# Values stored with their columns of ones, and a wait ahead of the second piece of keys

## The chip, the cores and the metric

The kernel runs on one core of one Trainium2 chip. The metric is the device time of one execution in microseconds; lower is better.

## The reference, cut to what matters

```python
B, N, C, n_agents, d_ff = 2, 12480, 128, 49, 2048
def sm(a, b):
    s = scale * (a @ b.transpose(0, 2, 1))
    e = np.exp(s - s.max(-1, keepdims=True))
    return e / (e.sum(-1, keepdims=True) + 1e-09)
agent_v = sm(agents, k) @ v                  # (B, 49, 128)
x = (sm(q, agents) @ agent_v).reshape(B * N, C)
h = x @ w_in                                 # (24960, 2048)
out = (np.maximum(h, 0.0) + alpha * np.minimum(h, 0.0)) @ w_out
```

Agents attend to all keys, queries attend to the agents, and a two-layer network with a leaky activation follows. All inputs are float32.

## The kernel before, in words

Five engines follow programs written out by hand, and semaphores alone order them. SyncE (SP in the rows) issues nearly all transfers, in the order of its program: where it waits, every later transfer waits too.

**Before the main loop** the keys and values of batch 0 are gone through. The keys come as a short tail tile `k_tail` and 12 full pieces of 1024 keys (`load_keys`, 512 KB each, one row of 4096 bytes a partition) into eight slots of `kv_s`. A slot has 4 * 257 + 1 = 1029 numbers a partition. TensorE scores each piece against the agents (`piece_scores`, line 480; 16 matmul records a piece), ScalarE saves the scores into `S`, VectorE takes maxima. Then GpSimd subtracts the maximum and ScalarE takes exp, piece by piece. After that TensorE multiplies the exps with the values (`first_values`, line 557; again 16 records a piece). The values come as 12 pieces of 8 tiles of 128 x 128 (`load_values`, line 289) into the same slots, once the keys there have been used.

A matmul of exps with 129 columns, one of them ones, gives the weighted sum and the denominator together. So a slot holds, for each pair of tiles, a one and then 256 numbers of values, and a last one at its end (RUN = 257). In the kernel before, the values lie in device memory without ones. The transfer puts four runs of 1024 bytes into each partition, between the ones (`without_ones`), and VectorE writes the ones (memsets on lines 1307, 1327, 1335 and 1388). TensorE waits for them (`ones_in`, `second_ones`).

**Behind the values** TensorE scores `k_tail` of batch 1, sums denominators, scores `first_keys` (first keys of batch 1), and turns the agents' values into mixed weights. From about 60 us on a loop over 49 chunks of 512 queries runs the network (lines 650, 667 and 677), and the keys and values of batch 1 are worked in between (`second_values` from chunk 12 on, six loads of 1 MB, `load_second`).

The order of SyncE's queue in the first 50 us: `k_tail`, six pieces of keys, `w_out`, six pieces of keys, `w_inT`, `w_in`, the first queries, `v_tail`, value piece 1, queries, value pieces 2 to 12, `k_tail` of batch 1, `first_keys`, queries, and then the transposes of the first chunk (PT<-stack). Value piece 1 waits for key piece 8 to be scored, value piece 5 for all keys, value piece m over 8 for value piece m - 8 to be used.

Of the kernel before, what the change touches and what calls it, by code (L numbers as in the profile page):

```python
# [11 lines left out]
B, N, C, A, F = 2, 12480, 128, 49, 2048  # L12
# [40 lines left out]
def build(nc, kT, kTail, vP, vS, vTail, qT, agT, w_in, w_inT, w_out, alpha_col, out):  # L53
    ctx = ExitStack()
    with ctx:
# [3 lines left out]
        def sem(name):  # L59
            return ctx.enter_context(nc.semaphore(name))  # L60
# [108 lines left out]
        in_q = [sem("in_q0"), sem("in_q1")]  # L169
        stored = [sem("stored0"), sem("stored1")]  # L170

        consts, stack_zero, ones_in, second_ones = sem("consts"), sem("stack_zero"), sem("ones_in"), sem("second_ones")
        pool_step, dve_step = sem("pool_step"), sem("dve_step")
        sel_ready, signs, lin_w_in, relu_w_in = sem("sel_ready"), sem("signs"), sem("lin_w_in"), sem("relu_w_in")
        signs_out, w_signed = sem("signs_out"), sem("w_signed")
# [72 lines left out]
        def value_slot(m):  # L248
            return (m + RING - 1) % (2 * RING)
# [3 lines left out]
            at = t // 2 * RUN + t % 2 * VC  # L253
            return slice(at, at + VC)


        def without_ones(x):
            return x.rearrange("p (j c) -> p j c", c=RUN)[:, :, 1:RUN]

        second_s = kv_s[:, RING:2 * RING, :].rearrange("p s c -> p (s c)")  # L260
        SECOND_SLOT = SECOND // 2 * RUN + 1

# [7 lines left out]
        @block.sync  # L270
        def _(sp):
            def load_keys(m):
                s = (m - 1) % KEY_SLOTS
                if m > KEY_SLOTS:

                    sp.wait_ge(k_scored, m - KEY_SLOTS + 1)
                sp.dma_start(kv_s[:, s, 0:PIECE], kT[0, m - 1]).then_inc(in_k[s], 16)

            def load_values(m):
                if m == 1:  # L280

                    sp.wait_ge(k_scored, KEY_SLOTS + 1)
                if m == RING + 1:

                    sp.wait_ge(k_scored, FULL + 1)
                if m > 2 * RING:

                    sp.wait_ge(v_used, m - 2 * RING + 1)
                sp.dma_start(without_ones(kv_s[:, value_slot(m), 0:4 * RUN]),
                             vP[m - 1].rearrange("p (j c) -> p j c", c=2 * C)).then_inc(in_v[(m - 1) % (2 * RING)], 16)  # L290

            def load_tail(b):
                sp.dma_start(v_tail[:, b, 1:RUN], vTail[b]).then_inc(in_vt[b], 16)

            sp.dma_start(k_tail[:, 0, :], kTail[0]).then_inc(in_kt[0], 16)
            for m in range(1, FULL + 1):
                load_keys(m)
                if m == 6:
                    sp.dma_start(w_lin[:, :, :], w_out).then_inc(in_wo, 16)
            sp.dma_start(w_inT_s[:, :, :], w_inT).then_inc(in_wT, 16)  # L300
            sp.dma_start(w_in_s[:, :], w_in).then_inc(in_wn, 16)
            sp.dma_start(q_s[:, 0, :], qT[0]).then_inc(in_q[0], 16)
            load_tail(0)
            load_values(1)
            sp.dma_start(q_s[:, 1, :], qT[1]).then_inc(in_q[1], 16)
            for m in range(2, FULL + 1):
                load_values(m)

            sp.dma_start(k_tail[:, 1, :], kTail[1]).then_inc(in_kt[1], 16)
            sp.dma_start(first_keys[:, :], kT[1, 0]).then_inc(in_first, 16)  # L310

            def load_queries(n):

                sp.wait_ge(q_scored, n - 1)
                sp.dma_start(q_s[:, n % 2, :], qT[n]).then_inc(in_q[n % 2], 16)

            load_queries(2)

            def load_second(half, j):
                sp.dma_start(without_ones(second_slot(half)[:, 0:SECOND // 2 * RUN]),  # L320
                             vS[j].rearrange("p (j c) -> p j c", c=2 * C)).then_inc(in_second[half], 16)


            def turn(n, half, read=None):

                parts = n - 1
                if not isinstance(n, int):
                    parts = sp.compute_val(parts)

                sp.wait_ge(stack_zero, 1)  # L330
                if read is not None:

                    sp.wait_ge(lin_ready, parts)
                sp.wait_ge(q_hi, n + 1)
                sp.wait_ge(q_dup, n + 1)
                sp.wait_ge(q_lo, n + 1)
                for t in range(4):
                    sp.dma_start(PT[:, half, t * WIDE:(t + 1) * WIDE], stack[:, t, :], transpose=True).then_inc(q_turned, 16)

            def spread(n, half):  # L340

                sp.wait_ge(q_turned, 64 * n + 64)
                for g in range(32, 128, 32):
                    sp.dma_start(PR[g:g + 32, half, :], PT[0:32, half, :]).then_inc(q_spread, 16)

            turn(0, 0)
            load_queries(3)
            spread(0, 0)

            sp.wait_ge(v_used, 2 * RING + 1)  # L350
            for h in range(2):
                sp.dma_start(kv_s[:, h, 0:PIECE], kT[1, EARLY + h - 1]).then_inc(in_k[h], 16)
            load_tail(1)
            turn(1, 1)
            spread(1, 1)

            def body(i, b, kind):
                for half in range(2):
                    n = 2 * i + half
                    if not there(n):  # L360
                        break
                    if there(n + 4):

                        sp.wait_ge(q_scored, n + 3)
                        sp.dma_start(q_s[:, half, 0:width(n + 4)], qT[n + 4][:, 0:width(n + 4)]).then_inc(in_q[half], 16)
                    if kind == KEYS and (not isinstance(n, int) or n + 2 + EARLY <= FULL):

                        sp.wait_ge(k_scored, n + (FULL + EARLY + 2))
                        sp.dma_start(kv_s[:, half, 0:PIECE], kT[1, n + (EARLY + 1)]).then_inc(in_k[half], 16)
                    if kind == TOP:  # L370

                        sp.wait_ge(v_used, FULL + 1)
                        load_second(half, half)
                    if kind == VALUES and (not isinstance(n, int) or n + 2 - FIRST_VALUES < SECONDS):

                        sp.wait_ge(v_used, n + (FULL + 2 - FIRST_VALUES))
                        load_second(half, n + (2 - FIRST_VALUES))
                    if there(n + 2):
                        turn(n + 2, half, n)
                        spread(n + 2, half)  # L380
                    if there(n + 1):

                        sp.wait_ge(y_ready, n + 1)
                        sp.dma_start(out[n], y[:, half, :]).then_inc(stored[half], 16)
                    else:

                        sp.wait_ge(last_y, 1)
                        sp.dma_start(out[n][:, 0:LAST // 2], y[:, half, 0:LAST // 2]).then_inc(stored[half], 16)

            each_body(sp, body)  # L390

            sp.wait_ge(stored[0], 16 * BODIES + 16)
            sp.wait_ge(stored[1], 16 * BODIES + 16)
# [83 lines left out]
        def _(pe):  # L477
# [63 lines left out]
            def first_values(m):  # L541
# [2 lines left out]
                    pe.wait_ge(in_vt[0], 16)  # L544
                else:
                    pe.wait_ge(in_v[(m - 1) % (2 * RING)], 16 * ((m - 1) // (2 * RING) + 1))

                pe.wait_ge(ones_in, RING + 1 if m <= RING else 2 * RING + 1)
                pe.wait_ge(k_exped, m + 1)
                for t in range(count):  # L550
                    if m == 0:
# [252 lines left out]
            def body(i, b, kind):  # L804
                for half in range(2):
# [33 lines left out]
                        pe.wait_ge(in_k[half], 16 * i + 16 * (FULL // KEY_SLOTS + 2))  # L839
                    if kind == VALUES:  # L840
                        pe.wait_ge(in_second[half], 16 * i + 16 * (1 - FIRST_VALUES // 2))

                        pe.wait_ge(second_ones, 2)

                        pe.wait_ge(k_exped, n + (FULL + 2 - FIRST_VALUES))
                        second_values(half)
# [300 lines left out]
        def _(dve):  # L1147
# [156 lines left out]

            dve.memset(stack[:, :, :], 0.0).then_inc(stack_zero, 1)

            dve.memset(v_tail[:, :, 0:RUN + 1:RUN], 1.0).then_inc(ones_in, 1)

            dve.wait_ge(consts, 4)
            for g in (0, 64):  # L1310
                for at, lo, hi in ((0, 0, A), (A, 0, A), (2 * A, REST, A), (128, 0, REST)):
# [3 lines left out]
            for m in range(FULL + 1):  # L1315
# [4 lines left out]
                if m == 9:  # L1320
                    dve.wait_ge(relu_w_in, 1)
                    dve.tensor_reduce(w_col[:, 0:1], w_relu[:, :, :], AX.XY, ALU.max,
                                      apply_absolute_value=True).then_inc(relu_col, 1)
                if m == KEY_SLOTS:

                    for s in range(RING, KEY_SLOTS):
                        dve.memset(kv_s[:, s, 0:4 * RUN + 1:RUN], 1.0).then_inc(ones_in, 1)
            key_max_column(0)
            relu_max_top()
            key_max_diagonal(0, K_BANK)  # L1330
            key_max_save(0, K_BANK)

            dve.wait_ge(k_scored, FULL + 1)
            for s in range(RING):
                dve.memset(kv_s[:, s, 0:4 * RUN + 1:RUN], 1.0).then_inc(ones_in, 1)
            weight_scale()
            query_shift(0)

# [39 lines left out]
            def body(i, b, kind):  # L1378
                for half in range(2):
# [2 lines left out]
                        break  # L1382
                    g = 2 * PAIRS * i + PAIRS * half
                    if kind == TOP and half == 0:

                        dve.wait_ge(v_used, FULL + 1)
                        for h in range(2):
                            dve.memset(second_slot(h)[:, 0:SECOND_SLOT:RUN], 1.0).then_inc(second_ones, 1)

                        dve.wait_ge(b_turned, 1)  # L1390
                        dve.memset(av_rows[:, :], 0.0).then_inc(av_added, 1)
# [106 lines left out]
```

## Time and profile before

| | us |
|---|---|
| median of 3 runs | 900.53 (900.29 to 901.55) |
| the profiled execution, its own time | 901.17 |
| its span in the trace | 899.4 |
| TensorE busy | 892.1, 99% of the span |
| VectorE busy | 619.2, 69% |
| ScalarE busy | 502.4, 56% |

The span is the stretch from the first to the last instruction; the execution's own time has 1.8 us more around it. PE is TensorE's matmuls, PEld its weight loads, DVE is VectorE, ACT is ScalarE, POOL is GpSimd, SPq is SyncE's queue. TensorE is busy nearly all the time, so what matters are its few idle stretches, and who ends them.

### The profile page before, as it was taken

What the parts mean: (1) busy time and instruction counts of PE and PEld (TensorE: products, weight loads), DVE (VectorE), ACT (ScalarE), POOL (GpSimd) and SP (SyncE); (2) the same over time, 40 slices, a digit from 0 to 9 for tenths busy, and PEclk for the clock granted to TensorE, in tenths of its full rate; (3) what the DMA queues carried; (4) which work ended last, traced back from release to release, by engine and by line L of the source; (5) the groups of instructions that cost most, each with busy time, mean ns of one, the idle gap of its engine ahead of it and who ended that gap; (6) DMA issues with size and microseconds to landing.
All of it is one profiled execution on the core that took longest, in us unless ns stands there. A gap on an engine that the chain in (4) does not pass through costs nothing.

```text
span 899.4 us, 15332 instructions
## 1 busy us (share of the span) xinstructions
PE 892.1 (99%) x5496; PEld 451.9 (50%) x5496; DVE 619.2 (69%) x883; ACT 502.4 (56%) x653; POOL 105.5 (12%) x130
## 2 busy tenths in 40 slices
PE   9999999999999999999999999999999999999998
PEld 9855555555544545444444444444444444444444
DVE  4877767766776667678666676667667676766664
ACT  2445565555555555565555566556565655665554
POOL 6500010001000100010001001011010010010100
PEclk9999999999999999999999999999999999999999
DMA  9952223122322341111112112111111121121110
GB/s 358 359 155 82 62 64 103 58 63 69 98 83 85 98 130 43 39 45 53 36 39 62 35 40 61 35 41 58 38 42 54 39 56 38 39 61 33 30 36 21
DMA packets 69975, 66.13 MB, mean 74 GB/s; under 512 B 36368, under 2 KB 54192, under 8 KB 69552
## 3 DMA queue, kind: packets, MB, share of 16 engines
q1 hardware_dynamic: 69504, 65.45, 23.9%
q8 instruction: 25, 0.41, 0.2%
q10 hardware_dynamic: 432, 0.16, 0.1%
q14 instruction: 14, 0.11, 0.0%
HBM read 41.54 MB, written 12.78 MB: 60 GB/s over the span
## 4 chain that ended last, share of the span: by engine, by line
PE 96%; DMA 2%; DVE 1%; ACT 0%; issue 0%; SPq 0%; DVEq 0%; ACTq 0%
PE ps L677 57%; PE ps L650 18%; PE ps L667 7%; PE ps L618 3%; PE ps L480 2%; PE ps L868 2%; PE ps L565 1%; PE ps L692 1%; DMA kv_s<-vP 1%; DVE r_lo L1296 1%; PE ps L595 1%; PE ps L557 1%; DMA kv_s<-kT 1%; PE ps L703 1%; PE ps L510 0%; ACT r_hi L1041 0%
## 5 line engine op out<-in xcount | busy, mean ns | idle before, releaser
L1296 DVE SCALAR_TENSOR_TENSOR r_lo<-ps,r_hi 128x1024 f16<-128x1024 f32 (+1 forms) x392 | 468.3, 1215 | 247.2 <-ACT r_hi L1041 246.8
L1041 ACT ACTIVATE r_hi<-ps 128x1024 f16<-128x1024 f32 (+1 forms) x392 | 388.6, 1017 | 261.0 <-PE ps L667 254.7
L677 PE MATMUL ps<-r_hi,w_hi 128*128 128x512 f16 (+1 forms) x784 | 244.5, 380 | 0.1
L677 PE MATMUL ps<-r_hi,w_lo 128*128 128x512 f16 (+1 forms) x784 | 241.3, 378 | 0.0
L677 PE MATMUL ps<-r_lo,w_hi 128*128 128x512 f16 (+1 forms) x784 | 234.2, 378 | 0.0
L650 PE MATMUL ps<-PT,M_a 128*128 128x512 f16 x768 | 197.6, 379 | 0.4 <-DVE r_lo L1296 0.3
L462 POOL TENSOR_TENSOR y<-y_relu,y_lin 128x512 f32<-128x512 f32 x48 | 60.7, 1266 | 599.6 <-ACT y_relu L1137 404.1
L677 PEld LDWEIGHTS ps<-r_hi,w_lo 128*128 128x128 f16 x784 | 84.5, 109 | 76.0
L677 PEld LDWEIGHTS ps<-r_lo,w_hi 128*128 128x128 f16 x784 | 78.9, 104 | 78.0
L650 PEld LDWEIGHTS ps<-PT,M_a 128*128 128x128 f16 x768 | 74.7, 98 | 81.3 <-DVE r_lo L1296 2.4
L677 PEld LDWEIGHTS ps<-r_hi,w_hi 128*128 128x128 f16 x784 | 66.7, 104 | 87.3 <-issue 40.0
L667 PE MATMUL ps<-PR,M_r 32*128 32x512 f16 x576 | 75.1, 385 | 0.0
L667 PE MATMUL ps<-PT,M_r 32*128 32x512 f16 x192 | 73.8, 384 | 0.0
L618 PEld LDWEIGHTS ps<-agents,q_s 128*128 128x128 f32 x384 | 66.6, 190 | 10.2 <-issue 0.2
L618 PE MATMUL ps<-agents,q_s 128*128 128x49 f32 x384 | 60.5, 243 | 0.0
L667 PEld LDWEIGHTS ps<-PT,M_r 32*128 32x128 f16 x192 | 17.3, 90 | 81.4 <-issue 81.0
L1033 ACT ACTIVATE stack<-q_p 128x196 f16<-128x196 f32 x49 | 18.3, 373 | 61.1 <-DVE q_p L1287 58.8
L1137 ACT ACTIVATE y_relu<-ps,out_unscale 128x512 f32<-128x512 f32 x48 | 33.0, 687 | 33.8 <-PE ps L677 33.8
L443 POOL TENSOR_TENSOR stack<-stack,ones 128x120 f16<-128x120 f16 x49 | 19.6, 400 | 163.8 <-ACT stack L1033 163.8
L1114 ACT ACTIVATE y_lin<-ps,lin_unscale 128x512 f32<-128x512 f32 x48 | 32.7, 682 | 0.0
L868 PEld LDWEIGHTS ps<-agents,kv_s 128*128 128x128 f32 x176 | 30.8, 191 | 2.6 <-DVE M_a L1246 0.4
L1161 DVE TENSOR_REDUCE k_top<-S 128x49 f32<-128x392 f32 (+2 forms) x26 | 19.9, 775 | 12.2 <-ACT S L997 12.2
(166 smaller groups left out, 491.2 us busy)
## 6 DMA issues: line engine op xcount, KB each, us to landing
q_s<-qT SPq DMA_DIRECT2D x48, 256.0 KB, 2.8
out<-y SPq DMA_DIRECT2D x48, 256.0 KB, 2.1
kv_s<-kT SPq DMA_DIRECT2D x23, 512.0 KB, 4.5
kv_s<-vP SPq DMA_DIRECT2D x12, 512.0 KB, 8.9
kv_s<-vS SPq DMA_DIRECT2D x6, 1024.0 KB, 6.1
PR<-PT SPq DMA_DIRECT2D x147, 32.0 KB, 1.9
PT<-stack SPq DMA_TRANSPOSE x196, 2.4
w_lin<-w_out SPq DMA_DIRECT2D x1, 1024.0 KB, 10.2
```

The costliest lines, as they stand in the source:

```text
L443: pool.tensor_tensor(stack[0:T, :, 2 * A:128], stack[0:T, :, REST:A], ones[0:T, 0:4 * SPARE].rearrange("p (t a) -> p t a", a=SPARE), ALU.m ...
L462: pool.tensor_tensor(y[:, half, :], y_relu[:, half, :], y_lin[:, half, :], ALU.add).then_inc(y_ready, 1)
L618: return pe.matmul(ps[0:T, SMALL, t * A:(t + 1) * A], q_s[:, half, t * T:(t + 1) * T], agents[:, b * A:(b + 1) * A], start=True, stop=True)
L650: pe.matmul(by_tile(ps[:, 2 * slot(p) + u, 0:CHUNK]), M_a[:, b, f:f + 128], tokens(PT, half), start=True, stop=False)
L667: mm = pe.matmul(by_tile(ps[:, 2 * slot(2 * q + u // 2) + u % 2, 0:CHUNK]), M_r[32 * u:32 * u + 32, b, q * 128:(q + 1) * 128], tokens(src[ ...
L677: mm = pe.matmul(ps[:, OUT, 0:wide], w[:, 2 * p + u, :], r[:, s, u, 0:wide], start=(p == 0 and u == 0 and k == 0), stop=(p == PAIRS - 1 an ...
L868: mm = pe.matmul(ps[:, SMALL, t * A:(t + 1) * A], kv_s[:, half, t * KT:(t + 1) * KT], agents[:, A:2 * A], start=True, stop=True)
L1041: act.activation(r_hi[:, p % RING, :, 0:wide], ps[:, at:at + 2, 0:wide], ACT.Relu).then_inc(hi_ready, 1)
L1114: act.activation(y_lin[:, half, :].rearrange("p (h n) -> p h n", n=HALF), ps[:, 2 * LIN_SLOT:2 * LIN_SLOT + 2, 0:HALF], ACT.Copy, scale=li ...
L1137: act.activation(y_relu[:, half, :], ps[:, OUT, 0:CHUNK], ACT.Copy, scale=out_unscale[:, b, :]).then_inc(relu_saved, 1)
L1161: dve.tensor_reduce(k_top[:, b, m, :], by_agent(piece(b, m)), AX.X, ALU.max).then_inc(k_maxed, 1)
L1296: dve.scalar_tensor_tensor(out=r_lo[:, p % RING, :, 0:wide], in0=ps[:, at:at + 2, 0:wide], scalar=0.0, in1=r_hi[:, p % RING, :, 0:wide], o ...
```

## The change

The host lays the values out with the ones already between them, so that the values of a piece are one row of 1029 numbers (4116 bytes) a partition, in place of four runs of 1024 bytes. The same holds for the loads of batch 1 (2057 numbers a row in place of eight runs) and for the tails (258 in place of 256 numbers). The memsets of the ones and TensorE's waits for them go. Apart from that, SyncE waits for `k_tail` to land before it issues the second piece of keys.

```diff
@@ load_keys
                     sp.wait_ge(k_scored, m - KEY_SLOTS + 1)
+                if m == 2:
+                    sp.wait_ge(in_kt[0], 16)
                 sp.dma_start(kv_s[:, s, 0:PIECE], kT[0, m - 1]).then_inc(in_k[s], 16)
@@ load_values, load_tail, load_second
-                sp.dma_start(without_ones(kv_s[:, value_slot(m), 0:4 * RUN]),
-                             vP[m - 1].rearrange("p (j c) -> p j c", c=2 * C)).then_inc(in_v[(m - 1) % (2 * RING)], 16)
+                sp.dma_start(kv_s[:, value_slot(m), :], vP[m - 1]).then_inc(in_v[(m - 1) % (2 * RING)], 16)
-                sp.dma_start(v_tail[:, b, 1:RUN], vTail[b]).then_inc(in_vt[b], 16)
+                sp.dma_start(v_tail[:, b, :], vTail[b]).then_inc(in_vt[b], 16)
-                sp.dma_start(without_ones(second_slot(half)[:, 0:SECOND // 2 * RUN]),
-                             vS[j].rearrange("p (j c) -> p j c", c=2 * C)).then_inc(in_second[half], 16)
+                sp.dma_start(second_slot(half), vS[j]).then_inc(in_second[half], 16)
@@ TensorE, first_values and the body of VALUES
-                pe.wait_ge(ones_in, RING + 1 if m <= RING else 2 * RING + 1)
-                        pe.wait_ge(second_ones, 2)
@@ VectorE
-            dve.memset(v_tail[:, :, 0:RUN + 1:RUN], 1.0).then_inc(ones_in, 1)
-                if m == KEY_SLOTS:
-                    for s in range(RING, KEY_SLOTS):
-                        dve.memset(kv_s[:, s, 0:4 * RUN + 1:RUN], 1.0).then_inc(ones_in, 1)
-            dve.wait_ge(k_scored, FULL + 1)
-            for s in range(RING):
-                dve.memset(kv_s[:, s, 0:4 * RUN + 1:RUN], 1.0).then_inc(ones_in, 1)
-                        dve.wait_ge(v_used, FULL + 1)
-                        for h in range(2):
-                            dve.memset(second_slot(h)[:, 0:SECOND_SLOT:RUN], 1.0).then_inc(second_ones, 1)
@@ on the host
+    def between_ones(x):
+        runs = np.ones(x.shape[:-2] + (x.shape[-2] // 2, RUN), x.dtype)
+        runs[..., 1:] = x.reshape(x.shape[:-2] + (x.shape[-2] // 2, 2 * C))
+        runs = runs.reshape(x.shape[:-2] + (-1,))
+        return np.concatenate([runs, np.ones(x.shape[:-2] + (1,), x.dtype)], axis=-1)
```

SyncE's queue at the start of the kernel before (kT, w_out and vP are arrays in device memory; "waits" names semaphores that the instruction waits for):

```order
L295 DMA k_tail<-kTail 128x192
L277 DMA kv_s<-kT 128x1024 x6
L299 DMA w_lin<-w_out 128x2048
L277 DMA kv_s<-kT 128x1024 x2
L277 DMA kv_s<-kT 128x1024 [waits k_scored] x4
L300 DMA w_inT_s<-w_inT 128x2048
L301 DMA w_in_s<-w_in 128x2048
L302 DMA q_s<-qT 128x512
L293 DMA v_tail<-vTail 96x256
L289 DMA kv_s<-vP 128x4x256 [waits k_scored]
```

The same place of the queue with the change:

```order
L293 DMA k_tail<-kTail 128x192
L276 DMA kv_s<-kT 128x1024
L276 DMA kv_s<-kT 128x1024 [waits in_kt0]
L276 DMA kv_s<-kT 128x1024 x4
L297 DMA w_lin<-w_out 128x2048
L276 DMA kv_s<-kT 128x1024 x2
L276 DMA kv_s<-kT 128x1024 [waits k_scored] x4
L298 DMA w_inT_s<-w_inT 128x2048
L299 DMA w_in_s<-w_in 128x2048
L300 DMA q_s<-qT 128x512
L291 DMA v_tail<-vTail 96x258
L288 DMA kv_s<-vP 128x1029 [waits k_scored]
```

No transfer changes its place; the second piece of keys has a wait ahead of it, with all that is behind it, and a value piece is one run of 1029 numbers a partition where it was four of 256.

VectorE's program where the maximum of the keys is done, in the kernel before:

```order
L1179 COPY k_shift<-ps 128x49 [waits b_top]
L1335 MEMSET kv_s 128x5 [waits k_scored]
L1335 MEMSET kv_s 128x5 x3
L1192 COPY w_max<-ps 128x1 [waits relu_all]
L1193 RECIPROCAL w_scale<-w_max 128x1 [waits dve_step]
```

And with the change:

```order
L1172 COPY k_shift<-ps 128x49 [waits b_top]
L1185 COPY w_max<-ps 128x1 [waits relu_all]
L1186 RECIPROCAL w_scale<-w_max 128x1 [waits dve_step]
```

The four memsets between the copy of the maximum and the scale of the weights are gone; nothing else there moves.

## Rows read from the trace of the kernel before

**Rows 1.** The page: span, TensorE, and the chain that ended last, by engine

```profile
span 899.4 us, 15332 instructions
PE 892.1 (99%) x5496; PEld 451.9 (50%) x5496; DVE 619.2 (69%) x883; ACT 502.4 (56%) x653; POOL 105.5 (12%) x130
PE 96%; DMA 2%; DVE 1%; ACT 0%; issue 0%; SPq 0%; DVEq 0%; ACTq 0%
```

**Rows 2.** The chain, 0 to 8 us: start, duration, what

```profile
1.73 5.72 DMA kv_s<-kT
7.44 0.04 issue
```

**Rows 3.** The timeline of TensorE, 2 to 9 us: start, duration, group

```profile
4.18 0.93 PE L710 MATMUL ps<-ones 128*128 128x128 f32 x6
4.99 2.03 PE L480 MATMUL ps<-agents,kv_s 128*128 128x98 f32 x16
```

**Rows 4.** The chain, 0 to 130 us: keys scored, then the last value wait

```profile
7.49 19.89 PE ps L480 x176
40.30 8.62 DMA kv_s<-vP
```

**Rows 5.** The chain, 20 to 50 us: three value pieces in a row

```profile
35.87 2.78 PE ps L557 x48
```

**Rows 6.** The timeline of TensorE, 41 to 51 us: the last six value pieces

```profile
41.81 2.29 PE L557 MATMUL ps<-kv_s,S 128*49 128x129 f32 x32
44.04 0.38 PE L539 MATMUL ps<-w_diag,ones 2*128 2x2 f32 x2
44.50 1.09 PE L557 MATMUL ps<-kv_s,S 128*49 128x129 f32 x16
46.00 1.09 PE L557 MATMUL ps<-kv_s,S 128*49 128x129 f32 x16 [0.41 <-DMA kv_s<-vP]
47.45 1.09 PE L557 MATMUL ps<-kv_s,S 128*49 128x129 f32 x16 [0.36 <-DMA kv_s<-vP]
48.96 1.09 PE L557 MATMUL ps<-kv_s,S 128*49 128x129 f32 x16 [0.42 <-DMA kv_s<-vP]
```

**Rows 7.** Transfers, 16 to 20 us, when only keys move

```profile
DMA packets 445, 1.63 MB, mean 409 GB/s; under 512 B 49, under 2 KB 49, under 8 KB 444
```

**Rows 8.** Transfers, 33 to 43 us, when only values move

```profile
DMA packets 3485, 3.48 MB, mean 348 GB/s; under 512 B 108, under 2 KB 3483, under 8 KB 3483
```

**Rows 9.** Transfers by issue: us to landing; k_tail, key pieces 1 and 7, v_tail, first_keys

```profile
DMA to landing us min/median/max: 2.2/2.2/2.2
...
kv_s<-kT SPq DMA_DIRECT2D x1, 512.0 KB, 3.7
...
kv_s<-kT SPq DMA_DIRECT2D x1, 512.0 KB, 10.8
...
v_tail<-vTail SPq DMA_DIRECT2D x1, 96.0 KB, 15.7
...
first_keys<-kT SPq DMA_DIRECT2D x1, 512.0 KB, 7.3
```

**Rows 10.** The timeline of SyncE: k_tail, keys 1 to 6, key 7, v_tail, first_keys issued

```profile
0.80 0.40 SPq L295 DMA_DIRECT2D k_tail<-kTail  x1
1.25 3.52 SPq L277 DMA_DIRECT2D kv_s<-kT  x6
5.52 0.49 SPq L277 DMA_DIRECT2D kv_s<-kT  x1
14.91 0.43 SPq L293 DMA_DIRECT2D v_tail<-vTail  x1
43.17 0.43 SPq L310 DMA_DIRECT2D first_keys<-kT  x1
```

**Rows 11.** The timeline of ScalarE, 41 to 55 us: last exp, then behind the values

```profile
43.03 0.53 ACT L1001 ACTIVATE S<-S 128x392 f32<-128x392 f32 x1 [0.38 <-POOL S L451]
```

**Rows 12.** The timeline of VectorE: memsets at 31 us, and work around the last value piece

```profile
31.33 0.09 DVE L1335 MEMSET kv_s<- 128x5 f32 x3
45.61 2.07 DVE L1263 SCALAR_TENSOR_TENSOR w_lo<-w_relu,w_scale,w_hi 128x512 f16<-128x512 f32 x3
50.10 0.15 DVE L1360 COPY den_col<-ps 49x1 f32<-49x1 f32 x1 [2.42 <-PE ps L557]
```

More of the change, by code:

```diff
@@ L170, in build @@
         stored = [sem("stored0"), sem("stored1")]
-        consts, stack_zero, ones_in, second_ones = sem("consts"), sem("stack_zero"), sem("ones_in"), sem("second_ones")
+        consts, stack_zero = sem("consts"), sem("stack_zero")
         pool_step, dve_step = sem("pool_step"), sem("dve_step")
@@ L254, in with_ones @@
             return slice(at, at + VC)
-        def without_ones(x):
-            return x.rearrange("p (j c) -> p j c", c=RUN)[:, :, 1:RUN]
         second_s = kv_s[:, RING:2 * RING, :].rearrange("p s c -> p (s c)")
@@ L1478 @@
         "kTail": k[:, full:].transpose(0, 2, 1),
-        "vP": v[0, :full].reshape(FULL, 8, KT, C).transpose(0, 2, 1, 3).reshape(FULL, KT, 8 * C),
-        "vS": v[1, :full].reshape(SECONDS, SECOND, KT, C).transpose(0, 2, 1, 3).reshape(SECONDS, KT, SECOND * C),
-        "vTail": v[:, full:].reshape(B, 2, TAIL, C).transpose(0, 2, 1, 3).reshape(B, TAIL, 2 * C),
+        "vP": between_ones(v[0, :full].reshape(FULL, 8, KT, C).transpose(0, 2, 1, 3)),
+        "vS": between_ones(v[1, :full].reshape(SECONDS, SECOND, KT, C).transpose(0, 2, 1, 3)),
+        "vTail": between_ones(v[:, full:].reshape(B, 2, TAIL, C).transpose(0, 2, 1, 3)),
         "qT": queries.transpose(0, 2, 1),
```

## The prediction

> **What bounds the kernel now.** I read the page first, for what the whole is bound by, then the chain of work that ended last for the places where it leaves TensorE, and then the timelines and the transfers of those places. TensorE is busy 892.1 of 899.4 us, and the chain is TensorE's for 96% [rows 1]. So a time saved or lost anywhere on TensorE's path before the main loop comes back one for one at the end, and nothing that only relieves VectorE or SyncE counts. The chain leaves TensorE for a transfer at two places only. One is the second piece of keys, issued at 1.73 and landed 5.72 later, at 7.44 [rows 2]; TensorE's first piece ended at 4.99 + 2.03 = 7.02 [rows 3], so 0.47 us are idle there. The other is the last value pieces: the chain goes through a value transfer from 40.30 to 48.92 [rows 4]. Pieces 9 to 12 start at 44.50, 46.00, 47.45 and 48.96, that is one in 1.49 us, and three of them have an idle stretch ended by the transfer [rows 6]. Three value pieces without such a wait take 2.78 us together, 0.93 each [rows 5]. So from piece 9 on the transfers set the pace, and TensorE would be faster by 0.56 us a piece.
>
> The transfers run without a gap from 2 us to the end of the values, but not at one rate. While keys move, rows of 4096 bytes, the core gets 409 GB/s [rows 7]; while values move, runs of 1024 bytes, 348 GB/s [rows 8]. A piece of 524 KB thus takes 1.28 us as keys and 1.51 us as values, which is the 1.49 us seen on TensorE. Same source memory, same 128 partitions, same slots: what differs is the run.
>
> **The change part by part: rows of 4116 bytes.** A value piece becomes one row a partition. That it then moves at the rate of the keys is read across from keys to values; no row of before shows a row of 4116 bytes, or one that starts off a round address in device memory. The bounds of its cost: below, the keys' rate, (4116 x 128 bytes) / 409 = 1.29 us a piece; above, nothing gained at all, 1.51 us. I take 1.29, because in the slots of `kv_s` the keys too start off round addresses (a slot is 4116 bytes) and still move at 409 GB/s; only the reading side is new.
>
> What that is worth at TensorE. Everything ahead of the values has landed when `v_tail` has, at 14.91 + 15.7 = 30.6 [rows 9, 10]. Behind it come 12 pieces at 1.29, 15.5 us, and one load of queries of 262 KB, 0.64 us at 409 GB/s: piece 12 lands at 30.6 + 15.5 + 0.6 = 46.7. When would TensorE want it? Piece 7 starts at 41.81 [rows 6]; pieces 7 and 8 take 1.86, the small matmul of line 539 0.35 more (0.38 with its tail), pieces 9 to 11 2.79: piece 12 could start at 46.8. Its exps are there, since ScalarE's last exp ends at 43.03 + 0.53 = 43.6 [rows 11]. So transfer and TensorE come out even, and piece 12 starts at 46.8 in place of 48.96: **-2.15 us**. The slots don't hold the loads back: a piece m over 8 waits for piece m - 8, and piece 4 is done by 38.65, the end of the three pieces at 35.87 + 2.78 [rows 5], 8 us before piece 12 is wanted.
>
> Who is late next? VectorE has three instructions of `weights_low` from 45.61 to 47.68, then waited 2.42 us for the last values [rows 12]. With piece 12 ending at 46.8 + 1.1 = 47.9 it is just free. `first_keys` landed at 43.17 + 7.3 = 50.5 [rows 9, 10], 1.6 us behind value piece 12, and TensorE took it up 1.7 us after piece 12 began; both move together. I book nothing for these, and 0.3 us of slack on each is all the cover there is.
>
> **The memsets and waits.** Eleven memsets, each well under 0.1 us: those at 31 us took 0.09 for three [rows 12], and VectorE works on nothing there that TensorE waits for at once, since TensorE is busy with other matmuls right through to 41.81 (the chain is TensorE's from 7.49 until the value wait [rows 4]). Booked at nothing; were the cover gone, at most 0.1 us each at 31 us and at the first chunk with values of batch 1. The six loads of batch 1 and the tails are not on the chain at all [rows 1].
>
> **The wait ahead of key piece 2.** `k_tail` lands at 0.80 + 2.2 = 3.0 [rows 9, 10]. So piece 2 is issued at about 3.1, 1.36 us later than now, and the four pieces, `w_out` and all that stand behind it on SyncE's queue move with it. Piece 1 needed 3.7 us from issue to landing [rows 9], with k_tail ahead and nothing older; piece 2 needed 5.72 [rows 2]. Bounds: with 3.7, piece 2 lands at 6.8, before piece 1 is done, and TensorE saves its 0.47 idle us; with 5.72 it lands at 8.8 and TensorE loses 1.36. Between them decides whether the transfer engines run dry. Piece 1 was issued at 1.25 and landed at 4.9 [rows 9, 10]; a transfer issued at 3.1 follows while piece 1 still moves, so hardly a gap opens. But a gain is capped as well: key piece 7 landed at 5.52 + 10.8 = 16.3 [rows 9, 10], and TensorE, at 19.89 / 11 = 1.81 us a piece from 7.49 on [rows 4], wanted it at 7.49 + 5 x 1.81 = 16.5. It can run ahead by 0.2 us there, no more, unless the whole stream is earlier. I take **0**, and keep -0.47 and +1.36 for the range.
>
> **The sum.** 901.17 - 2.15 + 0 = 899.0 for an execution like the profiled one. That one is 0.64 above the median of the runs shown, so against the median 900.53 - 2.15 = **898.4**.
>
> **A rule that speaks against it.** No row of before shows a row that starts off a round address in device memory. The Trainium skill, DMA: Bandwidth & Descriptors, section "How a descriptor splits into AXI transactions", says that a read which doesn't start on a 256-byte boundary fetches from the boundary below, and that the unused bytes cost beats. By that page's count a row of 4116 bytes takes up to 137 beats in place of 128, an estimate of 7% more than a key row; the sum would be -1.2 us and not -2.15. No run here shows it yet.
>
> **The rivals.** *(1) Off-boundary rows cost part of the gain.* If a value piece takes 1.40 us, the middle of 1.29 and 1.51, piece 12 lands at 30.6 + 16.8 + 0.6 = 48.0 and starts there: -0.95 us, 899.6. For it: the reading side is untested; against it: the writing side shows no such cost. *(2) Rows off the boundary move slower than four runs do.* The point from which this makes the kernel slower is a row of 4116 bytes that takes longer than the four runs of now, 1.49 us a piece. If it is as much slower than the four runs as keys are faster, 1.51 + 0.22 = 1.73 us, piece 12 lands at 30.6 + 20.8 + 0.6 = 52.0 and starts 3.0 us later: 903.6. Nothing in the rows shows such a price, only that the case isn't covered. *(3) The key stream gains too.* Piece 2 needed 2 us more than piece 1, though the bytes ahead of it and its own are only some 1.2 MB, and others came between; with fewer transfers in flight it could land by 7.0 and the stream with it: -0.47 more, 897.9. *(4) The late issue leaves a gap.* The full 1.36 us at 8.8 is carried by all later keys and by the transfers; with -2.15 it leaves -0.8, 899.7. *(5) The change gives nothing*, because the rate falls for a reason of the place in the program and not of the run: 900.5. Against it: two stretches of 4 and 10 us at steady 409 and 348.
>
> **How the numbers follow.** Chances: forecast 0.42 (own range 898.0 to 898.8); rival 3 0.20; rival 1 0.18; rival 4 0.10; rival 5 0.05; slower by rival 2 or by 2 and 4 together 0.05. What a measurement of this kernel can tell from no change is about 0.2%, 1.8 us: faster is below 898.7, slower above 902.3. The forecast is only 0.3 us past that line, so I count 0.37 of its 0.42 as faster, with 0.20 of rival 3: 0.57, and 0.01 from rival 1. Within 0.2% are the rest of the forecast and rivals 1, 4 and 5. The range from 897.5 to 900.4 takes in the forecast and rivals 1, 3 and 4, about 0.85.
>
> **What would show each step.** Right: value pieces 9 to 12 start 0.93 us apart with no idle stretch ended by a value transfer; the rate while values move is near 409 GB/s, with some 3.2 times fewer packets; piece 12 begins near 46.8. Wrong in the rows: the pieces stay more than 1.1 us apart, and transfers still end TensorE's waits. For the keys: where piece 2 begins (now 7.49) and whether later key pieces, the seventh above all, have an idle stretch before them. The prediction fails if a new wait stands between 48 and 57 us (VectorE's `weights_low`, `first_keys`, the transposes) or if pieces of keys come late one after another.

## The result and the profile after

| | median us | runs |
|---|---|---|
| before | 900.54 (899.73 to 902.0) | 20 |
| changed | 898.94 (898.42 to 901.39) | 20 |

The ratio is 0.9984, 95% interval 0.9978 to 0.9990: 1.6 us faster, less than the 2.15 forecast. The profiled execution of the changed kernel took 899.25 us, with a span of 897.5.

The same views as before, of the changed kernel. First the page: span, engines and the chain by engine.

```profile
span 897.5 us, 15316 instructions
PE 892.1 (99%) x5496; PEld 453.3 (51%) x5496; DVE 619.3 (69%) x872; ACT 502.4 (56%) x653; POOL 105.6 (12%) x130
PE 98%; DVE 1%; ACT 0%; issue 0%; POOL 0%; DVEq 0%; ACTq 0%; POOLq 0%
```

The 2% of the chain that transfers had [rows 1] are gone; TensorE's busy time is the same to 0.1 us. The transfers at the place of [rows 8], 33 to 43 us:

```profile
DMA packets 1109, 4.07 MB, mean 407 GB/s; under 512 B 125, under 2 KB 125, under 8 KB 1107
```

348 GB/s have become 407, in a third of the packets (1109 for 3485); the keys' rate [rows 7] was 409. The chain of the changed kernel from 2 to 50 us (start, duration, what):

```profile
3.74 0.65 PE ps L477 x4
4.39 1.33 PE ps L705 x6
5.72 22.11 PE ps L477 x192
...
40.12 1.90 PE ps L552 x32
42.02 0.31 PE ps L532 x2
42.33 1.90 PE ps L552 x32
44.23 0.31 PE ps L536 x2
44.54 3.66 PE ps L552 x64
48.20 0.51 PE ps L477 x4
```

No transfer stands in it. Value pieces 9 to 12 (44.54 and 64 records) take 3.66 us, 0.92 each, where they stood 1.49 apart [rows 6]. The values end at 48.20, 1.85 us earlier than the 50.05 of before, though the keys end 0.45 later, at 5.72 + 22.11 = 27.83 against 27.38 [rows 4]. So two things are to be explained: the later keys, and why the median gains less (1.6 us) than this pair of traces (1.85).

In the forecast, value piece 12 and TensorE came out even. Here is its transfer as the changed kernel issued it, at 39.14 us (KB, us to landing):

```profile
kv_s<-vP SPq DMA_DIRECT2D x1, 514.5 KB, 6.7
```

It landed at 45.86, 1.3 us before TensorE started on it at 47.15. In two more traces of the changed kernel, shown below, the piece was 1.7 and 0.9 us early.

### The profile page after: what moved, and what is told of

Its sections match the earlier page's. It is cut to its first block, busy times and chain, and to the rows that moved or that the text cites. A ratio compares the mean times of both kernels' runs of the same rounds, so it can differ in the third digit from the quotient of the medians.

```text
span 897.5 us, 15316 instructions
## 1 busy us (share of the span) xinstructions
PE 892.1 (99%) x5496; PEld 453.3 (51%) x5496; DVE 619.3 (69%) x872; ACT 502.4 (56%) x653; POOL 105.6 (12%) x130
## 4 chain that ended last, share of the span: by engine, by line
PE 98%; DVE 1%; ACT 0%; issue 0%; POOL 0%; DVEq 0%; ACTq 0%; POOLq 0%
PE ps L672 57%; PE ps L645 18%; PE ps L662 7%; PE ps L613 3%; PE ps L477 3%; PE ps L861 2%; PE ps L552 1%; PE ps L560 1%; PE ps L687 1%; DVE r_lo L1289 1%; PE ps L590 1%; PE ps L698 1%; PE ps L705 0%; PE ps L507 0%; ACT r_hi L1034 0%; PE ps L642 0%
```

## The experiments

The experiments were run in three groups, each on one chip together with the kernel before, whose medians were 900.35, 900.49 and 900.42 us. Times of one group stand beside each other best. An interval is the 95% interval of the ratio to the kernel before. One trace was taken of each experiment; "the keys end" and "the values end" tell where TensorE is done with them in it. Except where it is said otherwise, a diff is against the changed kernel.

**Without the wait.**

```diff
-                if m == 2:
-                    sp.wait_ge(in_kt[0], 16)
```

> The changed kernel without SyncE's wait ahead of the second piece of keys: rows of 4116 bytes alone. Theory A (the rows give all of the gain, the wait nothing): within 0.3 us of the changed kernel, 898.9; value pieces about 0.93 us apart to the end. Theory B (the wait costs what the prediction missed): 898.4, 0.5 us faster than the changed kernel. Theory C (the wait itself gains): 899.3, 0.4 us slower, and the second piece of keys starts near 7.5 where the matmuls before it run 0.11 us apart.

898.51, 1.84 us under before; ratio 0.9981 (0.9973 to 0.9990). In its chain no transfer stands between the keys and the end of the values, and pieces 9 to 12 are 0.92 us apart:

```profile
5.35 21.41 PE ps L474 x192
...
43.48 3.66 PE ps L549 x64
47.13 0.51 PE ps L474 x4
```

**The wait alone**, added to the kernel before:

```diff
+                if m == 2:
+                    sp.wait_ge(in_kt[0], 16)
```

> The kernel before with the wait ahead of the second piece of keys and nothing else. Theory A: 900.5, as before. Theory B: 901.0. Theory C: no more than 0.1 us faster even so, since the values' transfers at 348 GB/s set the end of the value pieces whatever the keys do; value pieces 9 to 12 stay 1.49 us apart in all three.

900.84, 0.49 us over before; ratio 1.0005 (0.9996 to 1.0014), so the interval has "no change" in it (from 0.4 us gained to 1.3 us lost). Its value pieces are still paced by the transfers; the timeline of TensorE, 44 to 49.5 us:

```profile
47.13 1.09 PE L560 MATMUL ps<-kv_s,S 128*49 128x129 f32 x16 [0.36 <-DMA kv_s<-vP]
48.63 1.09 PE L560 MATMUL ps<-kv_s,S 128*49 128x129 f32 x16 [0.41 <-DMA kv_s<-vP]
```

So the rows give the gain. On the wait, both times lean to a loss (theory B), and against theory C.

**The changed kernel and the kernel before again**, unedited, in the same group.

> The changed kernel as it is, on the same chip as the others, for a second look at its start. Between 898.6 and 899.3. If matmuls stand 0.21 us apart until about 7 us again, the slow start belongs to the kernel; if the pace changes to 0.11 us at another time, it belongs to the execution, and the second piece of keys can start at about 7.1.

> The kernel before as it is, for a second look at its start. The matmuls' pace changes from 0.21 to 0.11 us apart near 4.4 us if that belongs to the kernel, and anywhere from 4 to 7.5 us if it belongs to the execution. Span 899 to 900.

The changed kernel took 899.13, 1.22 us under before (0.9986, 0.9978 to 0.9995); the one execution of the kernel before took 900.98, with a span of 899.3. The start belongs to the execution. Here is TensorE's timeline around 5 us (start, duration, group), first the six warm-up matmuls on `ones` and the keys in the first trace of the changed kernel:

```profile
4.18 1.54 PE L705 MATMUL ps<-ones 128*128 128x128 f32 x6
5.52 22.32 PE L477 MATMUL ps<-agents,kv_s 128*128 128x98 f32 x192
```

in its second trace:

```profile
4.18 0.90 PE L705 MATMUL ps<-ones 128*128 128x128 f32 x6
5.34 3.81 PE L477 MATMUL ps<-agents,kv_s 128*128 128x98 f32 x32 [0.26 <-DMA kv_s<-kT]
9.77 7.39 PE L477 MATMUL ps<-agents,kv_s 128*128 128x98 f32 x64 [0.62 <-DMA kv_s<-kT]
17.41 10.96 PE L477 MATMUL ps<-agents,kv_s 128*128 128x98 f32 x96 [0.25 <-DMA kv_s<-kT]
```

and in the second trace of the kernel before:

```profile
4.18 1.54 PE L710 MATMUL ps<-ones 128*128 128x128 f32 x6
```

The six matmuls took 0.93 us in the first trace of the kernel before [rows 3] and 1.54 in its second, 1.54 in the first of the changed kernel and 0.90 in its second. In the first trace of the changed kernel no piece of keys has to be waited for, but the matmuls are slow until about 7.1 us. In its second, three idle stretches are ended by a transfer of keys, among them the one before piece 7 (17.41), where the prediction saw 0.2 us of slack. In the second trace of the kernel before the keys ended at 27.31.

**A longer wait** (no wait for the short tile, but for the first piece of keys).

```diff
                 if m == 2:
-                    sp.wait_ge(in_kt[0], 16)
+                    sp.wait_ge(in_k[0], 16)
```

> Rows of 4116 bytes, and SyncE waits ahead of the second piece of keys for the first piece of keys to land (4.9 us) and not for the short tile (3.0): the wait of the change, 1.9 us longer. If a late issue costs by the gap that it leaves in the transfers, the rate from 5 to 6 us falls to under 200 GB/s, piece 2 lands near 8.7, and the time is 900.2 to 900.8, some 2 us above the kernel without a wait (898.5). If the wait was harmless and the changed kernel's 0.6 us above that kernel are chance of the start, 898.5 to 899.2.

900.60: 0.11 us over before (1.0003, 0.9994 to 1.0012), and 1.7 over the next experiment of this group, which has no wait (898.86; its interval, 0.9974 to 0.9992, doesn't meet this one). The stretches 4 to 5 and 5 to 6 us of this run (length, then the busy us of TensorE, its weight loads, VectorE, ScalarE and GpSimd, the granted clock, the share of the transfer engines, GB/s):

```profile
4.00:5.00 1.00, 1.00 (x7) 1.00 (x6) 0.26 (x1) 0.25 (x1) 0.00 (x0) 1.00 0.20 65
5.00:6.00 1.00, 1.00 (x8) 1.00 (x7) 0.00 (x0) 0.00 (x0) 0.68 (x4) 1.00 0.10 29
```

The second piece is issued at 4.8 and lands 3.6 later, as fast as piece 1 did [rows 9]. But for nearly two microseconds hardly anything moves, and the keys end at 29.19, 1.4 us later than in the next experiment (27.76). The same stretch, 4 to 5 us, in three traces of the changed kernel (the third is of the last group):

```profile
4.00:5.00 1.00, 1.00 (x7) 1.00 (x6) 0.26 (x1) 0.25 (x1) 0.04 (x1) 1.00 0.71 244
```

```profile
4.00:5.00 1.00, 1.00 (x9) 0.89 (x7) 0.26 (x1) 0.25 (x1) 0.00 (x0) 1.00 0.88 171
```

```profile
4.00:5.00 1.00, 1.00 (x7) 1.00 (x6) 0.26 (x1) 0.25 (x1) 0.14 (x1) 1.00 0.86 199
```

and in three of the kernel before:

```profile
4.00:5.00 1.00, 1.00 (x10) 0.93 (x8) 0.26 (x1) 0.25 (x1) 0.00 (x0) 1.00 1.03 277
```

```profile
4.00:5.00 1.00, 1.00 (x7) 1.00 (x6) 0.26 (x1) 0.25 (x1) 0.00 (x0) 1.00 1.01 352
```

```profile
4.00:5.00 1.00, 1.00 (x7) 1.00 (x6) 0.26 (x1) 0.25 (x1) 0.00 (x0) 1.00 0.84 195
```

On average 205 GB/s against 275, so some 70 KB are missing, 0.17 us at 409 GB/s. With the other experiments there are four traces with the short wait, 171 to 244 and 211 GB/s on average, and eight without any, 195 to 352 and 294 on average: 0.2 us. The scatter between executions is as large as the difference of the kernels.

**Rows that start on 256-byte boundaries** (without the wait; on the host the rows of batch 0 are padded to 1088 numbers, which the diff leaves out).

```diff
-                sp.dma_start(kv_s[:, value_slot(m), :], vP[m - 1]).then_inc(...)
+                sp.dma_start(kv_s[:, value_slot(m), :], vP[m - 1][:, 0:4 * RUN + 1]).then_inc(...)
```

> No wait; the rows of value pieces of batch 0 are padded in device memory to 1088 numbers, so that each starts on a 256-byte boundary; 1029 are loaded. If a start off the boundary costs anything, value pieces move at more than the 408 GB/s of the changed kernel and the time falls; since TensorE sets the pace of the values already, by no more than 0.1 us. If it costs nothing, 408 GB/s and 898.5.

898.86, 1.63 us under before (0.9983, 0.9974 to 0.9992), and over 33 to 43 us:

```profile
DMA packets 1109, 4.07 MB, mean 407 GB/s; under 512 B 125, under 2 KB 125, under 8 KB 1107
```

The same packets and the same rate as unpadded (1109, 407 GB/s). The start off the boundary costs nothing that can be seen.

**Three runs a partition** (without the wait; of every 344 numbers in device memory the first 343 are loaded; the host's part is left out of the diff).

```diff
-                sp.dma_start(kv_s[:, value_slot(m), :], vP[m - 1]).then_inc(...)
+                sp.dma_start(kv_s[:, value_slot(m), :].rearrange("p (j c) -> p j c", c=343),
+                             vP[m - 1].rearrange("p (j c) -> p j c", c=344)[:, :, 0:343]).then_inc(...)
```

> No wait and no memsets, but a value piece of batch 0 comes as three runs of 1372 bytes a partition in place of one of 4116. From 1.28 us a piece in 4096-byte rows and 1.49 in 1024-byte runs a run costs 9 ns and 0.037 ns a byte: 1.43 us a piece, 370 GB/s, the last pieces 1.4 us apart, 899.3 to 899.7. If freed memsets and waits gave the gain and not the run length, 898.5 and pieces 0.93 us apart.

899.90, 0.59 us under before (0.9996, 0.9987 to 1.0005), 0.2 us above what the run length foretold; its interval has "no change" in it, so the rate is the better witness. The rate from 33 to 43 us, foretold as 370 GB/s:

```profile
DMA packets 2771, 3.67 MB, mean 367 GB/s; under 512 B 111, under 2 KB 2769, under 8 KB 2769
```

and the last value piece waits for its transfer again (timeline of TensorE, 44 to 49.5 us):

```profile
44.49 2.92 PE L550 MATMUL ps<-kv_s,S 128*49 128x129 f32 x48
47.77 1.09 PE L550 MATMUL ps<-kv_s,S 128*49 128x129 f32 x16 [0.36 <-DMA kv_s<-vP]
```

348, 367 and 407 GB/s for runs of 1024, 1372 and 4116 bytes: the run sets the rate, with memsets and TensorE's waits gone in all but the first. The gaps between the runs are in the slot in the kernel before and in device memory here; either way there are more and shorter packets (3485, 2771 and 1109 in 10 us).

The keys of this trace, in its chain:

```profile
5.72 22.13 PE ps L475 x192
```

That is the line of the changed kernel (5.72, 22.11), from a kernel without the wait: so the 0.45 us by which the first trace's keys were later need no wait to explain them, only the slow first matmuls.

**Memsets and waits kept** (without the wait ahead of the keys). The diff is cut to one of the places; the others are put back likewise.

```diff
+            dve.wait_ge(k_scored, FULL + 1)
+            for s in range(RING):
+                dve.memset(spare[:, RING + s, 4:9], 1.0).then_inc(ones_in, 1)
             weight_scale()
```

> No wait, rows of 4116 bytes, and the eleven memsets and TensorE's waits for them are kept where they were, the memsets on a tile that nobody reads. If they cost nothing, 898.5, as without them; if they gave part of the gain, up to 0.4 us more, 898.9.

899.09, 1.40 under before (0.9988, 0.9979 to 0.9997), 0.23 us above the padded kernel beside it, which is inside both intervals. The chain of its trace settles more:

```profile
7.36 19.89 PE ps L475 x176
27.25 0.31 PE ps L522 x2
...
47.62 0.51 PE ps L475 x4
```

The values end 20.37 us behind the keys (47.62 - 27.25). In the changed kernel that stretch is 20.37 too (48.20 - 27.83), so the four memsets in it and TensorE's waits for them cost nothing. Five lie ahead of it, and the keys end no later than without them. The other two lie behind it, and from the end of the values to the end of the span this trace is as long as one without memsets, 849.4 us for 849.5 (the kernel without the wait).

**The last group: both again, before again, and another queue for the short tile.**

> The kernel with rows of 4116 bytes and no wait, again, beside the changed kernel on one chip. If the wait costs what its gap in the transfers shows (some 0.3 us), 898.4 to 898.9 and 0.2 to 0.6 us under the changed kernel of this call. If the first reading was chance, no more than 0.1 us apart.

> The changed kernel again, beside the kernel without the wait. 898.8 to 899.3. In the trace from 4 to 5 us the transfers move 170 to 250 GB/s, in the kernels without the wait 270 to 350.

898.83 without the wait (1.59 us under before, ratio 0.9983, 0.9974 to 0.9992), 899.01 with it (1.41 under, 0.9983, 0.9974 to 0.9992). The difference is 0.18 here and was 0.62 in the first group. From 4 to 5 us the transfers moved 264 GB/s without the wait and 199 with it; 270 to 350 was expected of kernels without it.

> The kernel before, a third look. Keys end at 26.7 to 27.5 us, by how soon the matmuls' pace changes and by stalled packets; the last value piece ends at 49.3 to 50.1 and follows the transfers, not the end of the keys: if the keys end 0.5 us earlier than in the first look, the last value piece doesn't end 0.5 us earlier unless its transfers do.

900.51. In this execution of the kernel before the keys ended at 28.17, not at 26.7 to 27.5, and yet the values ended earlier than in the first trace, 49.42 for 50.05. The chain from 2 to 50 us:

```profile
5.30 11.87 DMA kv_s<-kT
17.21 10.96 PE ps L480 x96
...
39.60 8.69 DMA kv_s<-vP
48.33 1.09 PE ps L557 x16
49.42 0.51 PE ps L480 x4
```

**The short tile on ScalarE's queue**, without the wait:

```diff
-            sp.dma_start(k_tail[:, 0, :], kTail[0]).then_inc(in_kt[0], 16)
+            act.dma_start(k_tail[:, 0, :], kTail[0]).then_inc(in_kt[0], 16)
             act.dma_start(a_col[:, :], alpha_col).then_inc(in_acol, 16)
```

> Rows of 4116 bytes, no wait, and the short tile of keys of batch 0 is issued on ScalarE's queue behind the agents, so that SyncE issues the first piece of keys at 0.80 and not at 1.25. If the keys' stage is bound by when its transfers start, keys end up to 0.45 us earlier and the time is 898.1 to 898.5. If it is bound by the pace of the first matmuls, the time is that of the kernel without the wait, 898.6; if the short tile is late on the other queue, TensorE starts its scores later than 3.5 us and up to 0.4 us are lost.

903.36, 2.9 us over before (1.0028, 1.0018 to 1.0039) and 4.5 over the kernel without a wait of the same group. My price for a late short tile was off by a factor of ten. The timeline of TensorE, 2 to 13 us:

```profile
6.63 0.94 PE L473 MATMUL ps<-agents,k_tail 128*96 128x98 f32 x4 [2.90 <-DMA k_tail<-kTail]
7.36 1.54 PE L701 MATMUL ps<-ones 128*128 128x128 f32 x6
8.70 4.55 PE L473 MATMUL ps<-agents,kv_s 128*128 128x98 f32 x24
```

Issued at 1.25 with the first 512 KB piece ahead of it, the 96 KB tile needs 5.2 us to land, where it needed 2.2 at the head [rows 9]. TensorE's program has its scores first, so all keys wait behind it: the first piece starts at 8.70 in place of 4.99 [rows 3]. The matmuls then stay slow until 12.3 us. In the chain:

```profile
8.90 23.10 PE ps L473 x192
...
52.38 0.51 PE ps L473 x4
```

The keys end at 32.01, and the values 20.37 us behind them, as in the changed kernel.

## Why the prediction was right in its range, and what was mis-sized

The measured median, 898.94, lies in the stated range of 897.5 to 900.4, but just outside the forecast's own range (898.0 to 898.8) and above the 898.7 below which 0.57 of the chance had been put.

**Rows of 4116 bytes.** The mechanism was right: the rate (407 for 409 GB/s), the pace (0.92 us a piece for 0.93), and no new wait behind. The rule that the prediction cites, from the Trainium skill, DMA: Bandwidth & Descriptors, section "How a descriptor splits into AXI transactions" (by it -1.2 us), didn't show here: rows on the boundary and off it gave the same rate and the same packets. Rivals 1 and 2 fall with that, rival 5 with the three runs.

**The term that was mis-sized is "piece 12 starts at 46.8 in place of 48.96": -2.15, where the traces show -1.6.** The step took what one execution showed for what the kernel does. In the kernel before, the last value piece follows its transfer; with rows of 4116 bytes it follows the keys. Here are the ends of keys and values in every trace, in us:

| | keys end | values end | values behind keys |
|---|---|---|---|
| before | 27.38 | 50.05 | 22.67 |
| before | 27.31 | 49.87 | 22.56 |
| before | 28.17 | 49.42 | 21.25 |
| before, with the wait | 28.05 | 49.72 | 21.67 |
| three runs | 27.85 | 48.86 | 21.01 |
| changed | 27.83 | 48.20 | 20.37 |
| changed | 28.37 | 48.74 | 20.37 |
| changed | 27.26 | 47.62 | 20.36 |
| without the wait | 26.77 | 47.13 | 20.36 |
| without the wait | 27.96 | 48.33 | 20.37 |
| padded rows | 27.76 | 48.13 | 20.37 |
| memsets kept | 27.25 | 47.62 | 20.37 |
| longer wait | 29.19 | 49.56 | 20.37 |
| short tile late | 32.01 | 52.38 | 20.37 |

With rows of 4116 bytes the values end 20.37 us behind the keys each time, to 0.01: TensorE alone decides. In the kernel before, late keys are made up for by values that need to wait less. The trace on which the sum rested had 2.30 us more than 20.37, and the third of the kernel before had 0.88. The forecast had the values end at 47.9 in place of 50.05. On average of three they end at 48.19, because the keys end at 27.82 and not at 27.38, in place of 49.78. So about half of the missing 0.55 us is on each side. The medians show the same 1.6 us; that they agree so well is in part luck, since the three traces of the kernel before are of executions that took 901.17, 900.98 and 900.51, all above the medians of their groups, and three traces are few. The prediction had noted that the first was 0.64 above its median, and took the term from it whole.

That transfer and TensorE would come out even (46.7 and 46.8) was wrong on the safe side: piece 12 landed at 45.86, 46.04 and 45.69, from 0.9 to 1.7 us before TensorE took it.

From the end of the values to the end of the span all fourteen traces have 849.3 to 849.5 us, with the three of the kernel before at 849.4 and the three of the changed kernel at 849.3. So at most 0.1 us comes from the loop, where memsets and a wait went and loads of 1 MB have longer rows. The prediction read from [rows 1] that those loads are not on the chain; that line's 2% can't show it, but the chain from 60 us on has no transfer in either kernel.

**The wait ahead of key piece 2**, booked at nothing. All differences have the sign of a loss: issue 1.35 us later costs 0.49 on the kernel before, and 0.62 and 0.18 on the new rows; issue 3.1 us later costs 1.7. Only the last is clear of the intervals; for the short wait a loss is not shown. In the changed kernel piece 2 itself wasn't late. It landed 3.7 to 4.0 us after its issue, near the lower bound and not at 5.7: at 7.05, 6.97 and 6.78, and in the kernel before at 7.44, 7.33 and 7.11. Over all traces it landed between 6.8 and 8.0 with the short wait and just so without any, and piece 7 between 15.9 and 17.4 with it and between 15.7 and 17.2 without. No delay stands out of that scatter. What the traces do show of a loss is the gap, 0.17 to 0.2 us; the reason given for nothing, that piece 2 follows while piece 1 still moves, holds but for that. After the longer wait the gap is nearly 2 us, piece 7 lands at 18.19, and the whole shift stays. Rival 3 (the wait gains) had piece 2 right, which landed at about 7.0 in the changed kernel, but no gain came of it; rival 4 (the late issue leaves a gap) has the sign, at less than half its price of 1.36.

## What to carry to other kernels

Compare rates of transfers between stretches of one trace before believing that memory is the limit: here the same source gave 348 or 409 GB/s, and only the length of the contiguous run differed. A wait on the critical path that one trace shows is the difference of two things that scatter by themselves; size it from where both streams stand in several executions, not from one. Cut the span where one stretch is the same in every trace: here 20.37 us and 849.4 us were, so all that was left to explain was where the keys end. An issue that was 1.35 us late cost 0.2 to 0.6 us by its point values, while the transfers kept moving at some 200 GB/s, and one that was 3.1 us late cost 1.7. The short tile that starts TensorE's program cost 4.5 us when it lost its place at the head of the transfers.

The fastest kernel seen is the changed one without its wait: 1.84 and 1.59 us under before in two groups, by point values ahead of the changed kernel in both, not beyond the intervals.

## What the runs showed that I had not expected

Six warm-up matmuls at 4.18 us took 0.93 us in one execution of the kernel before and 1.54 in another of the same kernel (0.11 and 0.21 us from one start to the next). The slow form lasted until 6.0 us in that one and until 7.1 in the first trace of the changed kernel, and it doesn't decide the time alone: the two executions of the kernel before ended their keys within 0.1 us of each other, because the fast one then waited for piece 2 [rows 2, 3]. The granted clock reads 1.00, the 2.4 GHz level, in both stretches, so the row doesn't tell of it; TensorE had been busy since 1.23 us in each. In the execution with the short tile on the other queue TensorE was idle for 2.90 us until 6.63, and the same six matmuls took 1.54 us from 7.36 on. What sets the moment of the faster pace is left open.
